# Taking both half-steps of a delta-rule recurrence through TensorE as one pair, in every second slot of a fused attention and MoE kernel

## The reference

```python
# 1. recurrence; k_n is k divided by its norm
for t in range(S):
    y[:, :, t] = einsum('bhd,bhde->bhe', q[:, :, t], state)
    v_old = einsum('bhde,bhd->bhe', state, k_n[:, :, t])
    state = state + beta * einsum('bhd,bhe->bhde', k_n[:, :, t], v[:, :, t] - v_old)
# 2. x = y as [3072, 384]
x = ((x @ w_a) * (x @ w_b)) @ w_out          # d_ff 1536
# 3. one expert of 8 for each token, chosen by argmax of x @ w_gate + bias
out[mask] = gate_w[mask] * (relu(x[mask] @ w1[e]) @ w2[e])
```

## Time and profile before

| | us |
|---|---|
| median of 3 runs | 1060.2 (1057.98 to 1061.77) |
| the profiled execution, its time | 1058.58 |
| the profiled execution, its span (first to last instruction) | 1056.8 |
| TensorE busy | 953.8 (90% of the span) |
| VectorE, ScalarE, GpSimd busy | 506.3, 281.9, 322.5 |
| mean granted TensorE clock | 0.943 of full speed |

### The profile page before, as it was taken

One profiled execution on the slowest core, in us unless ns is written; L12 is line 12 of the kernel. 1 busy time (PEld: TensorE's weight loads), 2 busy tenths in 40 slices (PEclk: granted clock), 3 DMA queues, 4 the chain that ended last, 5 costly groups with the idle time before them and its releaser, 6 DMA issues.

```text
span 1056.8 us, 26974 instructions
## 1 busy us (share of the span) xinstructions
PE 953.8 (90%) x10820; PEld 817.5 (77%) x10821; DVE 506.3 (48%) x1099; ACT 281.9 (27%) x529; POOL 322.5 (31%) x589
## 2 busy tenths in 40 slices
PE   2664899999999999999999999999956999999995
PEld 2653787887778887888888888888845999999995
DVE  4865665467546664567356643333382222222221
ACT  3021223223232323222223222232301322232221
POOL 1112133433233343434343434332401222222221
PEclk8656899999999999999999999999967999999998
DMA  8686357855675667666775565443547511181110
GB/s 253 223 227 182 91 165 219 236 169 176 181 230 172 196 203 213 203 181 185 211 196 171 179 200 174 146 139 120 163 145 259 172 38 37 45 281 39 40 42 24
DMA packets 151512, 172.44 MB, mean 163 GB/s; under 512 B 109664, under 2 KB 115938, under 8 KB 151409
## 3 DMA queue, kind: packets, MB, share of 16 engines
q0 software_dynamic: 32800, 114.65, 32.7%
q1 hardware_dynamic: 118608, 56.30, 21.2%
HBM read 101.70 MB, written 69.40 MB: 162 GB/s over the span
## 4 chain that ended last, share of the span: by engine, by line
PE 71%; DMA 14%; DVE 6%; issue 2%; ACT 2%; POOL 2%; SPq 2%; DVEq 0%; ACTq 0%; POOLq 0%
PE bank L527 19%; PE bank L529 17%; PE bank L528 17%; DMA work<-we_in 7%; DMA wbuf<-expert_split_scratch 3%; PE bank L571 2%; PE bank L487 2%; PE bank L693 2%; PE bank L497 2%; PE bank L473 2%; DVE work L1036 1%; ACT work L748 1%; PE bank L439 1%; PE bank L507 1%; DMA work<-wt_in 1%
## 5 line engine op out<-in xcount | busy, mean ns | idle before, releaser
L527 PE MATMUL bank<-wbuf,x_hi 128*128 128x512 f32 (+1 forms) x582 | 246.1, 423 | 3.5 <-DVE x_lo L1321 1.3
L528 PE MATMUL bank<-wbuf,x_hi 128*128 128x512 f32 (+1 forms) x582 | 231.2, 397 | 0.0
L529 PE MATMUL bank<-wbuf,x_lo 128*128 128x512 f32 (+1 forms) x582 | 230.8, 396 | 0.0
L1390 POOL DMA_DIRECT2D expert_split_scratch<-work x128 | 70.0, 547 | 396.4 <-DVE work L1036 382.7
L748 ACT ACTIVATE work<-bank 128x512 f32<-128x512 f32 (+1 forms) x169 | 93.1, 551 | 362.9 <-PE bank L529 293.6
L527 PE MATMUL bank<-wbuf,g_hi 128*128 128x392 f32 (+1 forms) x488 | 173.7, 356 | 12.3 <-DVE g_lo L1059 7.5
L529 PE MATMUL bank<-wbuf,g_lo 128*128 128x392 f32 (+1 forms) x488 | 166.5, 341 | 0.0
L528 PE MATMUL bank<-wbuf,g_hi 128*128 128x392 f32 (+1 forms) x488 | 165.9, 340 | 0.0
L1036 DVE TENSOR_TENSOR work<-work 128x384 fp32r<-128x384 f32 x128 | 71.2, 557 | 183.0 <-ACT work L748 182.8
L527 PEld LDWEIGHTS bank<-wbuf,x_hi 128*128 128x128 f32 x582 | 110.7, 190 | 29.4 <-issue 2.9
L529 PEld LDWEIGHTS bank<-wbuf,x_lo 128*128 128x128 f32 x582 | 111.0, 191 | 26.4
(11 more groups left out here) (143 smaller groups left out, 1197.8 us busy)
## 6 DMA issues: line engine op xcount, KB each, us to landing
expert_split_scratch<-work POOLq DMA_DIRECT2D x256, 192.0 KB, 3.3
work<-we_in POOLq DMA_DIRECT2D x128, 192.0 KB, 3.9
work<-a_in POOLq DMA_DIRECT2D x24, 896.0 KB, 7.3
wbuf<-expert_split_scratch SPq DMA_DIRECT2D x24, 768.0 KB, 6.0
work<-wm_in POOLq DMA_DIRECT2D x18, 384.0 KB, 5.0
inverse_in_scratch<-work SPq DMA_DIRECT2D x24, 256.0 KB, 2.8
work<-a_in SPq DMA_DIRECT2D x6, 768.0 KB, 6.2
x_scratch<-work SPq DMA_DIRECT2D x48, 96.0 KB, 2.5
```

Of the source, the lines that this page charges most:

```text
L527: pe.matmul(o, a_hi, w_hi, start=first, stop=False)
L528: pe.matmul(o, a_hi, w_lo, start=False, stop=False)
L529: return pe.matmul(o, a_lo, w_hi, start=False, stop=last)
L1390: pool.dma_start(ws_hi[e, c], s_hi[j % 2].bitcast(F32)).then_inc(s_hs[j % 2], 16)
```

## The change

Both half-steps of a chunk (p = 0 and 1) are taken through the recurrence together, in the even slots; the odd slots are dense, with the keys' products of a later pair. `slot(n)` becomes `even_slot(n)` and `odd_slot(n)` on all engines. Buffers hold both half-steps side by side, and PSUM is cut into four areas of two banks, one bank for each half-step. Half-step 1 is laid out so that its batches lie on the other half of the partitions by feature, and its tokens are turned by 32, so that its first 32-row block lies on partitions 32 to 63 and 96 to 127. VectorE and ScalarE operations take both half-steps in one instruction of twice the width.

```diff
-NAT, NHH, NLOAD = 4, 5, 2
-AHEAD = 2 * GROUP
+PAIRS = STEPS // 2
+AHEAD = 4
+        def feature_rows(p, h):
+            return h if p == 0 else CH - h
+        def output_rows(p, h):
+            return CH - h if p == 0 else h
@@ tensor
+            def r_products(c):
+                pe.wait_ge(S["row"], 16 * (c + 1))
+                if c == 0:
+                    pe.wait_ge(S["zero"], 1)
+                    pe.wait_ge(S["wgl"], 1)
                 else:
+                    pe.wait_ge(S["sadd"], c)
...
+            def qs_products(p, u):
+                e = slice(u * HD, (u + 1) * HD)
+                for h in HALF:
+                    f, o = feature_rows(p, h), output_rows(p, h)
+                    mm = pe.matmul(px[o:o + CH, p, e], queries_of(p, u, f), a_s[f:f + HD, p, e],
+                                   start=(u == 0), stop=False)
+            def across(c):
+                pe.wait_ge(S["ucp"], c + 1)
+                pe.wait_ge(S["tw"], 32 * (c + 1))
+                pe.wait_ge(S["kqm"], c + 1)
                 for u in range(U):
                     e = slice(u * HD, (u + 1) * HD)
+                    for p in range(2):
+                        for h in HALF:
+                            r = slice(h + p * Q, h + p * Q + Q)
+                            o = slice(h + Q - p * Q, h + CH - p * Q)
+                            mm = pe.matmul(pr[o, p, e], a_t12[r, p, u * Q:(u + 1) * Q], a_u[r, p, e],
+                                           start=True, stop=True)
+                    if c >= 1:
+                        qs_products(0, u)
...
+            def even_slot(n):
+                c, t = n // 2, n - 1
+                r_products(c)
+                kq_products(c)
+                a_products(t, 0)
+                first_block(c)
+                b_products(t, 0)
+                across(c)
+                a_products(t, 1)
+                second_block(c)
+                b_products(t, 1)
+                y_and_s(c)
+                g_transposes(t, 0)
+                a_products(t, 2)
+                b_products(t, 2)
+                g_transposes(t, 1)
+                out_products(t, 0)
+                finish_tile(t, n)
+            def odd_slot(n):
+                t = n - 1
+                a_products(t, 0)
+                b_products(t, 0)
+                a_products(t, 1)
+                g_transposes(t, 0)
+                b_products(t, 1)
+                a_products(t, 2)
+                g_transposes(t, 1)
+                b_products(t, 2)
+                if n // 2 + AHEAD < PAIRS:
+                    kk_products(n // 2 + AHEAD)
+                out_products(t, 0)
+                finish_tile(t, n)
+            for c in range(AHEAD):
+                kk_products(c)
+            pe.wait_ge(S["small"], 48)
+            for i in range(PARTS):
+                gate_products(i)
             kq_products(0)
+            r_products(0)
+            first_block(0)
+            across(0)
+            second_block(0)
+            y_and_s(0)
+            x_transposes(0)
+            odd_slot(1)
@@ scalar
+            def odd_slot(n):
...
+                a_copy(t, 1)
+                g_split(t, 0)
...
+                hi_piece(n, 1)
+                a_copy(t, 2)
+                hi_piece(n, 2)
+                g_split(t, 1)
...
+                hi_piece(n, 3)
+                hi_piece(n, 4)
+                hi_piece(n, 5)
+                g_split(t, 2)
@@ gpsimd
+            pool.wait_ge(S["kk"], 2)
+            for i in range(10):
+                load_dense(i)
+            triangle(0)
+            load_row(0)
+            load_out_t(5)
+            load_out_t(6)
+            v_scale(0)
+            for i in range(10, 14):
+                load_dense(i)
             load_row(1)
+            for i in range(14, 16):
+                load_dense(i)
+            triangle(1)
+            for i in range(16, ND):
+                load_dense(i)
```

More of the change, by code:

```diff
@@ new lines, in first_block @@
+            def first_block(c):
+                if c == 0:
+                    pe.wait_ge(S["v2"], 1)
+                    pe.wait_ge(S["rq"], 1)
+                else:
+                    pe.wait_ge(S["rsub"], c)
+                pe.wait_ge(s_hh[c % 2], 16 * (c // 2 + 1))
+                for u in range(U):
+                    for p in range(2):
+                        for h in HALF:
+                            r = slice(h + p * Q, h + p * Q + Q)
+                            mm = pe.matmul(pr[r, p, u * HD:(u + 1) * HD],
+                                           a_hh[r, (2 * c + p) % GROUP, u * Q:(u + 1) * Q], values_of(p, u, r),
+                                           start=True, stop=True)
+                mm.then_inc(S["u1"], 1)
@@ L641, in _, with finish_tile @@
-            for n in range(AHEAD):
-                kk_products(n)
-            kq_products(0)
-            r_and_qs(0)
-            pe.wait_ge(S["small"], 48)
-            for i in range(FF // P // 2):
-                gate_products(i)
-            for n in range(STEPS + 1):
-                slot(n)
+            def finish_tile(t, n):
+                g_transposes(t, 2)
+                if n < STEPS:
+                    x_transposes(n)
+                out_products(t, 1)
+                out_products(t, 2)
@@ L868, in _ @@
             square(1)
+            for i in range(6, 10):
+                hi_dense(i)
+            gate_hi()
+            u_copy(0)
             sqrt(1)
-            hi_dense(6)
-            gate_hi()
-            for n in range(STEPS + 1):
-                slot(n)
+            y_copy(0)
+            x_split(0)
+            hi_dense(10)
+            hi_dense(11)
+            odd_slot(1)
+            for n in range(2, STEPS, 2):
+                even_slot(n)
+                odd_slot(n + 1)
+            odd_slot(STEPS)
             y2_copy(TILES - 1)
@@ L1171, in _ @@
             sub_steps(0, 1, 31)
-            r_sub(0)
-            dve.wait_ge(S["const"], 16)
+            gate_lo()
             kq_mask(0)
+            for i in range(6, 10):
+                lo_dense(i)
             norm_sum(1)
             norm_guard(1)
-            lo_dense(4)
-            lo_dense(5)
+            r_add(0)
+            w_form(0)
             norm_root(1)
-            gate_lo()
-            for n in range(STEPS + 1):
-                slot(n)
+            at_form(2)
+            at_form(3)
+            s_add(0)
+            x_split(0)
+            lo_dense(10)
+            lo_dense(11)
+            odd_slot(1)
+            for n in range(2, STEPS, 2):
+                even_slot(n)
+                odd_slot(n + 1)
+            odd_slot(STEPS)
             links = [0]
```

802 lines of the change are left out of this document (371 added, 431 removed).

## The result

The changed kernel takes **1121.2 us** (median of 4 runs, 1106.2 to 1122.5) against 1060.4 for the kernel before (1058.0 to 1061.8): ratio 1.056, 95% interval 1.051 to 1.060. It is slower by 61 us, where the forecast of 1021 had it faster by 39. The profiled execution took 1121.23 us, its span is 1119.3.

The account below looks back on a forecast made before the run. TensorE's executed work was taken as the bound, expert pieces in odd slots. Start-up 105, even slots 11 x 29.9, odd 267, slot 24 22.8 and stalls 5 gave 728.7 against 768.15, 39 us less: 1021 us, range 1005 to 1066.

Parts of the forecast that it names:

- the price of `across` and `second_block`: Even slots: 1.93 us a phase with one kind after the other; 1.24 if they fill each other's free blocks.
- rival 1: `across` and `second_block`: array emptied at each change between 32-row and 64-row matmuls, 0.13 us each, 43 us, giving 1064; chance 0.28.
- start of slot 2: Start-up: slot 2 starts at 105 instead of 129.5, 24.5 us earlier, the largest single term.
- even slots 2 to 22: Eleven slots taking both half-steps through the recurrence, 29.9 us each; 28.5 with the lower bound.
- odd slots 3 to 23: Dense slots bounded by expert pieces: eight of 24.5 us, three of 22.5, norm work 3.7; together 267 us.
- slot 24: Slot with dense work alone, forecast at 22.8 us; it took 22.16 before.
- stalls beside these: 5 us added for stalls of the kind that made a mean slot 28.0 instead of 27.32 us.
- Rival 2: Odd slots held longer by the expert chain (18 us, 1039), or slot 1 by its weights (1046); chance 0.14.
- rival 3: `first_block` and other 32-row phases: four 32-row blocks don't run together, 23 us more, 1044; chance 0.08.
- the dense part of a slot: TensorE's dense work in each even or odd slot, 20.7 us.
- the keys' products with kq: Even slots: 128 records together, 32 rounds of 58 ns and 0.33 us in and out, 2.19 us.
- the widened operations: VectorE and ScalarE work between phases, twice as wide, costed at nothing; without cover, 4 operations of 0.4 us.

Follow-up runs that it names:

- all_ungrouped: all_y_even with the 64-row queries' products put back behind each head's 32-row matmuls in `across` and `second_block`; 1055.5 us, ratio 0.996.
- Keys_fewer: Changed kernel with keys of pairs 2 and 3 loaded before w_out and 3 dense loads, not 10, before the first triangle; 1116.9 us.
- all_edits: Changed kernel with 32-row matmuls first in mixed phases, two odd-slot expert pieces behind the split, substitution steps before them, and Keys_fewer's start-up; 1030.7 us.
- all_y_even: all_edits with output-tile stores first on SyncE's queue and the last expert piece of even slots behind the last splits; 1004.6 us, ratio 0.947.
- grouped: Changed kernel with all 32-row matmuls ahead of the queries' products in `across` and `second_block`, one change of kind per phase; 1072.1 us, ratio 1.014.
- two_heads: Changed kernel with 32-row and 64-row matmuls alternating after every second head, 7 changes of kind per phase; 1082.8 us, ratio 1.027.

## Why the prediction was wrong

The step that failed is the price of `across` and `second_block`: "I take 1.93, between the bounds". The phase measured 3.93 us in the forecast's own count. With one change of kind it takes 2.08 (653.54 to 655.51, and 0.11 at the exit), so the forecast left out just the changes: 1.93 and 15 of 0.131 us are 3.90. That an even slot with one change in a phase takes 29.9 us, exactly the forecast's number, is in part luck: the two phases are 0.15 us longer each, and `y_and_s`, forecast at 2.19, took 1.90.

What the runs show in its place is rival 1, with its price: 0.13 us, taken from the gap between full and small blocks. The reason given against it, that the two kinds lie on other blocks, does not count: the blocks do not overlap here, and every change is paid. The Trainium skill states, in TensorEngine Tiling (Array Packing), section Key Properties, that a change of tiling mode, and not just of the tile, drains TensorE. The phases here agree, with 0.13 us as the price.

Rival 1 was given 0.28 and should have been the forecast: the one row that priced a change of block size and the one rule both spoke for it, and nothing measured spoke against. Its sum of 1064 is still 57 us short of 1121, so other terms failed too. By the forecast's own terms, against the profiled execution:

| term | forecast | measured | difference |
|---|---|---|---|
| start of slot 2 | 105 | 118.7 | 13.7 |
| even slots 2 to 22 | 328.9 | 397.5 | 68.6 |
| odd slots 3 to 23 | 267 | 288.1 | 21.1 |
| slot 24 | 22.8 | 25.7 | 2.9 |
| stalls beside these | 5 | in the rows above | -5 |
| end of slot 24 | 728.7 | 830.1 | 101.4 |

- **Even slots.** 11 x (33.63 - 29.89) = 41 us are the changes of kind. Of the other 28, waits are 6.9 (in slots 10, 12, 14 and 16), and some 21 are the lower clock level. The clock stood at the upper level throughout these slots before. For them it was in no term of the forecast and in no rival, and ten of its falls stand at the mixed phases themselves, so that rival 1 is dearer than its 43 us. Over slots 2 to 23 as a whole, all_ungrouped, which has the same phases and the same matmuls, tells waits and clock apart: busy time 641.9 against 616.1 and idle 43.7 against 4.1. So of 65.4 us the waits took 39.7, mostly in odd slots, and the lower clock 25.8.
- **Odd slots.** Rival 2's mechanism is there as well: 43 us of waits for `g_lo`, 14 times, the longest 6.8 us, and 36.8 us of idle time in the odd slots alone. Slots 3, 5, 7 and 9 took 28.8 to 30.6 us where 24.5 stood, in part because of the lower clock behind the wait (0.89 to 0.91 in these slots). The chain was followed rightly, but with a landing of 4.0 us; in slot 5 it is 7.01, in a stretch in which SyncE's queue issues its keys and a store of scaled products twice as wide. Slots 11 to 23 take 21.9 to 25.8, near the forecast. The chain is also not a bound: with its last two pieces behind the split, odd slots take 20.6 to 23.3 us.
- **Start-up.** The gate to slot 2 was wrong by 13.7 us. The keys came at 47.9, not 42, and the first dense product at 87.3, not 80. What was missed is the scaled products' store, which lands after 14 us among the dense loads; the forecast named that competition and let the substitution end at about its old time all the same (52; it ended at 57.9). The second miss is slot 1, 31.4 us from the first dense product to slot 2 and not 25. Keys_fewer and all_edits show that these weights hold slot 2 at 116 and 114 even when all ahead of it comes earlier. The forecast had the order right: the last two dense loads stand behind `triangle(1)` on GpSimd. But the triangle waits there 11.1 us for its load from DRAM, so that they are issued at 102.5 and land at about 105.9, not 94.
- **Right:** `first_block` on four blocks (rival 3 is false: 1.02 us for 1.00 forecast); the dense part of a slot; the keys' products with kq (2.22 us for 2.19, although the forecast's 0.33 us for the way in and out of `r_and_qs` should be 0.35 by its own numbers, 1.28 - 0.93); the widened operations of VectorE and ScalarE costed at nothing (no phase in slots 2 to 23 waits for `r_add` or `w_form` in the kernel after); the expert stage.

What the change does bring is then in all_y_even: pairs of 29.9 + 20.7 to 21.9 us instead of 54.6, and 1004.6 us, 5.3% below the kernel before and 16 below the forecast. Nearly all of it is lost when the heads' order is put back (ratio 0.996).

## What to carry to other kernels

Packing small matmuls onto free blocks of the array paid here among matmuls of one block size, and not across sizes; sort them by size within a phase, and count changes of size at 0.13 us each, and more if the clock falls at the end of a phase full of them. A rule and a row that agree outweigh an argument from geometry. When an engine's work is made coarser, look at each queue with a fixed order for what now stands behind a wait: three such places (conversions ahead of a split, steps behind a conversion, a store behind a load's wait) cost some 5 to 28 us each here by the medians, and were cheap to move.

## What was not expected of the hardware

- The price of a change between 32-row and 64-row matmuls is 0.13 us even where their blocks of the array do not overlap, and it is linear in their number (15, 7, 1).
- The clock falls without a wait. In slot 16 of all_ungrouped TensorE is busy all the time; behind a 3.7 us phase of small matmuls, full ones take 0.43 us from start to start instead of 0.23 (rows below). In all_y_even, with phases of 1.9 us, the two falls in slots 2 to 23 both come at waits. In the profiled executions of grouped and two_heads, too, no fall comes at a mixed phase without a wait beside it.

Two stretches of that slot (the first number behind the bracketed counts is the clock), and TensorE in order of time:

```profile
518.00:524.70 6.70, 6.70 (x124) 4.92 (x113) 1.95 (x3) 1.22 (x2) 1.60 (x3) 1.00 0.72 160
524.70:528.10 3.40, 3.40 (x18) 2.15 (x17) 0.25 (x1) 0.27 (x1) 0.00 (x0) 0.51 1.31 129
```

```profile
524.11 0.50 PE L566 MATMUL pab<-wbuf,x_hi 128*128 128x512 f32 x1
524.44 0.39 PE L567 MATMUL pab<-wbuf,x_hi 128*128 128x512 f32 x1
...
525.03 0.63 PE L566 MATMUL pab<-wbuf,x_hi 128*128 128x512 f32 x1
525.46 0.63 PE L567 MATMUL pab<-wbuf,x_hi 128*128 128x512 f32 x1
```
